# One attention and mixture-of-experts kernel: laying the two masked halves of each score row over each other before the softmax and the transposes

## The reference

```python
batch, n_heads, seq, head_dim = (4, 8, 576, 64)
def _attn_ref(q, k, v):                       # window = 64
    scores = scale * np.matmul(q, k.transpose(0, 1, 3, 2))
    rel = pos[:, None] - pos[None, :]
    scores = np.where((rel >= 0) & (rel < window), scores, -1000000000.0)
    scores = scores - np.max(scores, axis=-1, keepdims=True)
    attn = np.exp(scores)
    attn = attn / (np.sum(attn, axis=-1, keepdims=True) + 1e-09)
    return np.matmul(attn, v)
...
def _moe_ref(x, w1, w2, w3, w_out):           # 2304 rows, 512 -> 1024 -> 1024 -> 512
    return (((x @ w1) * (x @ w2)) @ w3) @ w_out
...
def _moe2_ref(x, w_gate, w_output_gate, w1, w2):  # 8 experts, top 1
    ...
```

## Time and profile before

| | |
|---|---|
| median of 3 runs | 713.54 us (713.48 to 714.02) |
| the profiled execution | 714.16 us, its span 712.4 us |
| mean granted TensorE clock | 0.998 |
| busy, share of the span | PE 99%, PEld 90%, DVE 45%, ACT 41%, POOL 17% |
| transposes of the attention (L593) | 144, 19.6 us busy |

### The profile page before, as it was taken

One profiled execution on the slowest core, in us unless ns is written; L12 is line 12 of the kernel. 1 busy time (PEld: TensorE's weight loads), 2 busy tenths in 40 slices (PEclk: granted clock), 3 DMA queues, 4 the chain that ended last, 5 costly groups with the idle time before them and its releaser, 6 DMA issues.

```text
span 712.4 us, 15049 instructions
## 1 busy us (share of the span) xinstructions
PE 704.9 (99%) x5147; PEld 644.7 (90%) x5148; DVE 323.2 (45%) x597; ACT 295.2 (41%) x699; POOL 123.8 (17%) x191
## 2 busy tenths in 40 slices
PE   8999999999999999999999999999999999999997
PEld 7999999999999999999999999888888888888885
DVE  5577554222154425431222668844456554652221
ACT  4577545322054435532212254445455444552221
POOL 6222011100021102010000001222222221222211
PEclk9999999999999999999999999999999999999999
DMA  9875220410011332106101043846265744511110
GB/s 327 272 261 186 69 59 24 137 57 1 30 46 53 102 114 68 38 24 230 51 1 45 1 138 127 288 144 207 92 217 187 233 163 140 179 35 44 32 44 30
DMA packets 44590, 80.13 MB, mean 112 GB/s; under 512 B 4413, under 2 KB 24893, under 8 KB 44544
## 3 DMA queue, kind: packets, MB, share of 16 engines
q1 hardware_dynamic: 39504, 64.01, 27.4%
q0 software_dynamic: 5040, 15.47, 6.3%
HBM read 70.03 MB, written 10.49 MB: 113 GB/s over the span
## 4 chain that ended last, share of the span: by engine, by line
PE 98%; DMA 1%; DVE 0%; ACT 0%; issue 0%; POOLq 0%; ACTq 0%; DVEq 0%
PE bank L483 28%; PE bank L485 27%; PE bank L484 27%; PE bank L606 3%; PE bank L577 3%; PE bank L763 3%; PE bank L593 2%; PE bank L741 1%; PE bank L496 1%; PE bank L723 1%; DMA w3r<-in_w3T 1%; PE bank L511 0%; PE bank L513 0%; PE bank L529 0%; PE bank L509 0%; PE bank L532 0%
## 5 line engine op out<-in xcount | busy, mean ns | idle before, releaser
L483 PE MATMUL bank<-Wh,abh 128*128 128x272 f32 (+1 forms) x288 | 83.4, 290 | 0.0
L485 PE MATMUL bank<-Wh,abl 128*128 128x272 f32 (+1 forms) x288 | 82.0, 285 | 0.0
L484 PE MATMUL bank<-Wl,abh 128*128 128x272 f32 (+1 forms) x288 | 81.8, 284 | 0.0
L1117 DVE TENSOR_TENSOR wbuf<-raw,wbuf 128x1024 f32 (+1 forms) x64 | 75.3, 1221 | 12.8 <-ACT wbuf L897 12.6
L1434 POOL TENSOR_TENSOR prob<-prob,rec 128x384 f32<-128x384 f32 x48 | 42.7, 911 | 176.9 <-DVE rec L1039 176.9
L1315 DVE TENSOR_TENSOR hTl<-bank,hTh 128x512 fp32r<-128x512 f32 x44 | 28.4, 686 | 96.1 <-ACT hTh L955 96.1
L483 PE MATMUL bank<-wbuf,hTh 128*128 (+1 forms) x176 | 70.7, 402 | 0.2 <-issue 0.2
L824 ACT ACTIVATE prob<-prob,nmx 128x128 f32<-128x128 f32 x144 | 55.9, 390 | 35.4 <-DVE nmx L1031 35.4
L483 PE MATMUL bank<-wbuf,xsTh 128*128 (+1 forms) x176 | 70.4, 400 | 0.0
L485 PE MATMUL bank<-wbuf,hTl 128*128 (+1 forms) x176 | 68.8, 391 | 0.0
L485 PE MATMUL bank<-wbuf,xsTl 128*128 (+1 forms) x176 | 68.6, 390 | 0.0
(11 more groups left out here) (213 smaller groups left out, 1444.1 us busy)
## 6 DMA issues: line engine op xcount, KB each, us to landing
raw<-in_expert_w SPq DMA_DIRECT2D x64, 512.0 KB, 4.4
qT<-in_qT SPq DMA_DIRECT2D x24, 192.0 KB, 3.1
kT<-in_kT SPq DMA_DIRECT2D x24, 192.0 KB, 3.4
x_rows<-x_sb POOLq DMA_DIRECT2D x18, 256.0 KB, 2.3
w3r<-in_w3T SPq DMA_DIRECT2D x8, 512.0 KB, 5.1
wo<-in_w_out SPq DMA_DIRECT2D x8, 256.0 KB, 8.1
woT<-in_w_outT SPq DMA_DIRECT2D x4, 512.0 KB, 8.4
vA<-in_v SPq DMA_DIRECT2D x16, 128.0 KB, 2.1
```

Of the source, the lines that this page charges most:

```text
L483: pe.matmul(dst, lh, rh, start=first, stop=False)
L484: pe.matmul(dst, lh, rl, start=False, stop=False)
L485: return pe.matmul(dst, ll, rh, start=False, stop=last)
L1117: dve.tensor_tensor(wbuf[:, bass.ds(wcol(e, part, 1, c * PC), PC)], raw[part * NP1 + c][:, :], f32(wbuf[:, bass.ds(wcol(e, part, 0, c * PC ...
```

## The change

Of the 128 keys in a block's window, query q (0 to 63) sees the last q + 1 down from itself, columns q + 1 to q + 64. So in each column c of 0 to 63, exactly one of columns c and c + 64 is visible. DVE masks the scores as before into one buffer `sm`, takes the larger of the two halves (`tensor_tensor` max, 128x192) into a tile that holds both heads of a pair beside each other, and reduces once per pair. ACT's six exponentials have 64 columns each; POOL's product is one of 128x384 per pair. PE makes three transposes for a pair, all into bank 4. `turn_out` moves from ACT to DVE: four products per pair, each of 64 partitions x 384 columns out of PSUM, by a triangle of ones and zeros (`side`), which puts each value back to the half it belongs to and zeros into the other. Its place in DVE's list is behind `Wl` or `abl` and in front of `masks`. Six of the eight subtractions for the low parts of w1 and w2 move from DVE to POOL, in the fold's steps.

```diff
             def turn(b, p):
                 G = b * NP + p
-                pe.wait_ge(masked, 2 * min(G + 2, (b + 1) * NP))
                 if G > 0:
                     pe.wait_ge(pt_ok, 2 * G)
-                if G > 0 and p == 0:
-                    pe.wait_ge(o_lo, G)
-                for h in range(2):
-                    pe.wait_ge(p_ok, 2 * G + h + 1)
-                    for i in range(3):
-                        mm = pe.transpose(turn_bank(p, h)[:, i * P:(i + 1) * P], prob[buf_of(p, h)][:, i * P:(i + 1) * P], ident[:, :])
-                    mm.then_inc(pt_done, 1)
+                pe.wait_ge(p_ok, G + 1)
+                for i in range(3):
+                    mm = pe.transpose(bank[4][:, i * P:(i + 1) * P], prob[p % 2][:, i * P:(i + 1) * P], ident[:, :])
+                mm.then_inc(pt_done, 1)
...
             def exps(b, p):
...
+                act.wait_ge(nmx_ok, b * NP + p + 1)
+                for i in range(6):
+                    pr, c = prob[p % 2][:, i * WIN:(i + 1) * WIN], p % 2 * 6 + i
+                    ex_i = act.activation(pr, pr, ACT.Exp, bias=nmx[:, c:c + 1], accum_out=sums[:, c:c + 1])
                 ex_i.then_inc(exp_ok, 1)
-
-            def turn_out(b, p, h):
-                act.wait_ge(pt_done, 2 * (b * NP + p) + h + 1)
-                act.activation(pT[buf_of(p, h)][:, :], turn_bank(p, h)[:, 0:3 * P], ACT.Copy).then_inc(pt_ok, 1)
...
             def masks(b, p):
+                G = b * NP + p
+                pr = prob[p % 2][:, :].rearrange("p (i h c) -> p i h c", h=2, c=WIN)
+                smv = sm[:, :].rearrange("p (i w c) -> p i w c", w=2, c=WIN)
                 for h in range(2):
-                    g, pr = 2 * (b * NP + p) + h, prob[buf_of(p, h)]
+                    g = 2 * G + h
                     dve.wait_ge(s_done, g + 1)
-                    dve.scalar_tensor_tensor(pr[:, :], score_bank(h)[:, 0:3 * P], SEQ_SCALE,
+                    if g > 0:
+                        dve.wait_ge(laid_ok, g)
+                    dve.scalar_tensor_tensor(sm[:, :], score_bank(h)[:, 0:3 * P], SEQ_SCALE,
                                              mask[:, 0:3 * P] if unit_of(p)[1] == 0 else mask[:, P:4 * P],
                                              ALU.mult, ALU.add).then_inc(masked, 1)
                     dve.wait_ge(masked, g + 1)
-                    dve.tensor_reduce(nmx[:, stat(p, h)], pr[:, :].rearrange("p (i c) -> p i c", c=P),
-                                      AX.X, ALU.max, negate=True).then_inc(nmx_ok, 1)
+                    dve.tensor_tensor(pr[:, :, h, :], smv[:, :, 0, :], smv[:, :, 1, :], ALU.max).then_inc(laid_ok, 1)
+                dve.wait_ge(laid_ok, 2 * G + 2)
+                dve.tensor_reduce(nmx[:, stats(p)], prob[p % 2][:, :].rearrange("p (g c) -> p g c", c=WIN),
+                                  AX.X, ALU.max, negate=True).then_inc(nmx_ok, 1)
+
+            def turn_out(b, p, h):
+                G = b * NP + p
+                rows = slice(h * WIN, (h + 1) * WIN)
+                lead = 0 if unit_of(p)[1] == 0 else 1
+                dve.wait_ge(pt_done, G + 1)
+                for w in range(2):
+                    keep = side[rows, (4 * w + lead) * WIN:(4 * w + lead + 3) * WIN].rearrange("p (i c) -> p i c", c=WIN)
+                    cut = dve.tensor_tensor(pT[buf_of(p, h)][w * WIN:(w + 1) * WIN, :].rearrange("p (i r c) -> p i r c", r=2, c=WIN),
+                                            bank[4][rows, 0:3 * P].rearrange("p (i r c) -> p i r c", r=2, c=WIN),
+                                            keep.unsqueeze(2).broadcast_to([WIN, 3, 2, WIN]), ALU.mult)
+                cut.then_inc(pt_ok, 1)
...
             def weight_splits(i):
-                if i in w12_steps:
-                    lo_w12(w12_steps.index(i))
+                if i in w12_steps[LATE:]:
+                    lo_w1(w12_steps.index(i))
...
                 own()
+                if i >= 2 and turned(i - 2) is not None:
+                    turn_out(0, turned(i - 2), 0)
+                    turn_out(0, turned(i - 2), 1)
                 if fold_scored(i) is not None:
                     masks(0, fold_scored(i))
...
+            def lo_w12(i):
+                wh, wl, wr, _, kt = w12[i]
+                ws = slice(kt * FF, (kt + 1) * FF)
+                pool.wait_ge(w12_hi, i + 1)
+                pool.tensor_tensor(wl[:, ws], wr[:, ws], f32(wh[:, ws]), ALU.subtract).then_inc(w12_lo, 1)
+
+            for i in range(len(w_order)):
+                if fold_weighed(i) is not None:
+                    normal(0, fold_weighed(i))
+                if i in w12_steps[:LATE]:
+                    lo_w12(w12_steps.index(i))
```

More of the change, by code:

```diff
@@ L102, in build @@
         vA, vB = put("vA", 2 * SFULL * P), put("vB", 2 * SFULL * P)
-        prob = [put(f"prob{i}", 3 * P) for i in range(4)]
+        sm = put("sm", 3 * P)
+        prob = [put(f"prob{i}", 3 * P) for i in range(2)]
         pT = [put(f"pT{i}", 3 * P) for i in range(4)]
-        mask = put("mask", 4 * P)
-        put("raw_room", PC - 2 * 3 * P)
+        mask, side = put("mask", 4 * P), put("side", 2 * 4 * WIN)
+        put("raw_room", P)
         attn_end = put.o
@@ L879, in _ @@
                 own()
-                if i >= 2 and turned(i - 2) is not None:
-                    turn_out(0, turned(i - 2), 0)
-                    turn_out(0, turned(i - 2), 1)
                 if i >= 2 and valued(i - 2) is not None:
@@ L900, in chunk @@
             def chunk(cc, c, batches, b, parity, final):
-                turns = lambda e: b is not None and turned(e) is not None
                 def hidden_tile(f):
@@ L939, in chunk @@
                     row_tile(i, n, tt)
-                    if turns(KF + i):
-                        turn_out(b, turned(KF + i), 0)
                     attend(KF + i)
@@ L1125, in attend @@
                 def attend(e):
+                    if b is not None and turned(e) is not None:
+                        turn_out(b, turned(e), 0)
+                        turn_out(b, turned(e), 1)
                     if b is not None and scored(e) is not None:
@@ L1406, in _ @@
             pool.sem_inc(const_ok, 1)
+            then(pool.memset(side[:, :], 1.0))
+            then(pool.memset(side[:, 4 * WIN:5 * WIN], 0.0))
+            for h in range(2):
+                for w in range(2):
+                    kept = side[h * WIN:(h + 1) * WIN, (4 * w + 1) * WIN:(4 * w + 4) * WIN].rearrange("p (i c) -> p i c", c=WIN)
+                    then(pool.affine_select(out=kept, in_=kept, compare_op=ALU.is_ge, fill=0.0, base=w - 1,
+                                            pattern=[[0, 3], [2 * w - 1, WIN]], channel_multiplier=1 - 2 * w))
             then(pool.memset(ones[:, :], 1.0))
```

39 lines of the change are left out of this document (14 added, 25 removed).

## The result

| | before | changed |
|---|---|---|
| median of 6 runs each | 713.60 us (713.22 to 714.13) | 743.34 us (741.42 to 746.45) |
| ratio | | 1.042, 95% interval 1.039 to 1.045 |
| the profiled execution, its span | 714.16, 712.4 | 746.4, 744.6 |
| mean granted clock | 0.998 | 0.979 |

The changed kernel is 29.7 us slower. The direction was forecast, the size was not: the forecast was 15.2 us, 728.7, and 743.3 lies above the range, which ended at 734. The profile is that of the execution of 746.4 us, the second longest of the six; the executions of 741.4 and 741.8 us had a mean granted clock of 0.986 and 0.988, this one 0.979.

A forecast was written before the change was run, and what follows sets the result against it. PE, busy 99% of the span, was taken as the bound, with little room in the loop DVE, ACT, DVE. Fold +11.8 and three chunks +3.4 gave +15.2 on the median 713.54: 728.7 us, range 714 to 734 (forecast's own 725 to 731).

The forecast's parts named there:

- 72 transposes at 0.11 us each: PE, three fewer transposes in each of 24 pairs: 7.9 us saved, 1.98 for each batch, all on the path.
- the price of a wait: PE: each new wait was counted as a loss in full, at its own length.
- The cut: DVE's four 64x384 products out of PSUM per pair: 0.52 us each, 2.08 a pair, bounds 0.24 and 0.57.
- rival 1: DVE: each cut starts only after the one before has ended, 0.57 us each, 732 us; chance 0.20.
- The overlap of the second mask with the maximum: DVE's masks: each maximum of 192 columns was priced at 0.39 us with hand-over, inside the masks' 2.55.
- GpSimd's subtraction: Fold: GpSimd's w2 subtraction of 1024 columns was to take 2.2 us and hold up DVE's w3 subtraction.
- The wait before the first row tile: Chunks with attention: PE waits 2.5 us for hidden tile 7's abl, early in the first row tile.
- before value(5) of the chunks: End of a chunk's batch: PE waits 0.6 us for o_lo(4), queued on DVE behind pair 5's cuts.
- The fold's 11.8: Steps to 79 us: DVE's longer loop makes PE wait, 10.3 or 12.0 us net; +11.8 taken.
- The pair's single maximum: DVE masks: one reduction after both heads, 2.55 us before the exponentials can begin, 1.37 later than before.
- 2 (no hold by GpSimd): Fold: GpSimd does not hold DVE up over a long subtraction; 724.5 us, 721 if cuts overlap fully; chance 0.20.
- Rival 3: DVE/ACT loops stay under PE's time, so the gain shows; 709.6 us at 0.24 a cut, 705.6 without waits; chance 0.12.

The follow-up runs named there:

- e10: Changed kernel with a maximum reduction and a signal for each head, exponentials in the order of the heads; 726.72 us.
- e4: Changed kernel with 24 unread products in front of PE's wait for tile 7's abl in the three chunks with attention; 738.33 us.
- e1: Changed kernel with a pair's four cuts reordered, both heads' lower half first, each reading the partitions it writes; 740.08 us.
- e11: Changed kernel with masks ahead of the cuts in DVE's list and a reduction and a signal for each head; 719.42 us.
- e9: Changed kernel with nearly all cuts moved to ACT copies and GpSimd products, w1/w2 subtractions on DVE, a reduction and signal for each head; 711.28 us.
- e12: Changed kernel with head 1's cuts on ACT and GpSimd, w1/w2 subtractions on DVE, a reduction and signal for each head; 712.65 us.
- e13: Kernel with ACT's copies, GpSimd's triangles and a signal for each head, plus the last pair's value placed later; 709.01 us.

## Why the prediction was wrong

**What held.** 72 transposes at 0.11 us each, shown where the clock is at its upper level (three take 0.33 in e10). The waits are in front of the places named, with the engine named. GpSimd holds DVE up. The rest of the kernel is unchanged but for 0.9 us, for which I have no cause; in most of the experiments it is within 0.5.

**The step that failed: the price of a wait.** "A wait that PE has not had until now is a loss in full" counted each wait at its length, and the work behind it at its old price. Behind the longest waits (3.26 us in the chunks, 4.07 before the fold's last value) the clock was granted at 0.50, and the work there took up to twice as long. With the measured prices of DVE and GpSimd and no clock effect, my own sum gives, as an estimate, about 14.2 for the fold and 2.2 a chunk: 20.7 in place of 15.2. Measured were 32.2. In the chunks 14.0 - 6.5 = 7.5 us are left, and e4, which fills these waits without shortening them, brings the chunks to 2.5 above before, 6.6 us less in the three. So there the missing term is shown to be the clock; e1's chunks, of one program and one wait, say the same with 1.5 us. In the fold 3.1 us are left, and 2.3 of them stand in one stretch of the same work: 5.19 us in place of 2.93 at a clock of 0.50 from the last value to the first score. No run filled the fold's waits. (PE's slower work is 14.2 us in all and more than what is left of the sum, since in the fold, where DVE is late anyway, a slower PE waits less.)

**Terms mis-sized.** The cut: 0.52 taken, 0.57 measured, which is 3.4 us by the forecast's own slopes; e1 shows the hold behind it. That was rival 1, whose 732 was right in mechanism and too small for the same missing term. The overlap of the second mask with the maximum (0.39 taken, 0.46 measured) and GpSimd's subtraction (2.2 taken, 2.4 measured) make most of the other 2.1. The wait before the first row tile: 2.5 taken, 3.26 measured; before value(5) of the chunks: 0.6 taken, 0.94 measured. The fold's 11.8 stood between the sums 10.3 and 12.0 without a working of its own.

**A term right in size and not seen for what it was.** The pair's single maximum, "1.37 later", stood in the sum. Its part of the loop is 1.0 us, and undoing it alone gives 16.6 us, since it repeats in each loop, adds up over two loops of a chunk, and because behind the shorter waits of the chunks the clock stays up. The prediction never priced it as a choice of its own. With it undone and the cuts left in front of the masks, the kernel still takes 726.72, 13 us more than before; with the cuts behind the masks and it left as it is, 721.64. Undoing the order alone gives 21.7, so the effects don't add (16.6 and 21.7, and 23.9 together in e11): each edit takes away most of the same waits and slow work in the chunks.

**Rivals.** 2 (no hold by GpSimd) and 3 (loops under PE's time) fall for the changed kernel. Rival 3's mechanism is what e9, e12 and e13 show once cuts and exponentials stand elsewhere.

## What to carry to other kernels

When work moves to an engine with idle time, write down the loop that runs through it and the other engines, and put in it what is queued in front of the next link; a busy share of 50% says nothing. Look for the place in the list where the moved work stands beside another engine's turn instead of in front of it, and keep the early signal (one for each head) even if it costs an instruction. Price a wait of PE with the work behind it at the lower clock if the trace shows the clock fall behind waits like it, and look at what fills it: even useless products there gave 5 us back. Where one execution keeps its clock behind a wait and another doesn't, a single profile can mislead by microseconds: read it beside the median and the clocks of the other executions.

## What the runs showed of the hardware that wasn't expected

- PE's granted clock was 0.50 in the work behind the waits of 3.26 us (all three chunks of the changed kernel) and of 4.07 and 4.09 us (its fold and e10's); the products there have a pitch of 0.23 us in place of 0.13. 24 useless products in the wait kept it at 1.00. The length of one wait doesn't decide it alone: behind 2.65 to 2.67 us (e1) it stayed at 1.00 in two chunks and fell in one, behind 2.27 us in e10's fold it stayed, behind 2.29 us in the changed kernel's it fell (0.50 from 51.4 to 54.8), and in e9 it was 0.51 from 76.5 to 79.9, behind a wait of 1.70. What else decides it was not tried.
- DVE's products of 64 x 384 out of PSUM take 0.55 us each (0.537 to 0.564), like those of 128 x 384. Their pitch is 0.57 when the partition ranges change and 0.47 when they don't.
- ACT copies 64 x 384 from PSUM into another half of the partitions in 0.49 us, as long as 128 x 384. GpSimd's product of 128 x 384 by a broadcast triangle takes 1.02 us, by a broadcast column 0.83.
